# A fused attention, MoE and MLP kernel: the gate factor goes with the scattered rows, and the token order is made once

## The reference

```python
# 1: clustered attention, B=2, H=8, S=768, D=64, 16 clusters
mask = q_assign[:, :, :, None] == k_assign[:, :, None, :]
attn = softmax(where(mask, q @ k.T / sqrt(D), -1e9)); attn_out = attn @ v
x = attn_out.transpose(0, 2, 1, 3).reshape(1536, 512)
# 2: mixture of experts, E=8, F=1024, one expert for a token
logits = x @ w_gate;  e_idx = argmax(logits, axis=1)
gate_w = exp(logits - max)[e_idx] / (sum(exp(logits - max)) + 1e-09)
eom = 1.0 / (1.0 + exp(-(x @ w_output_gate)))
for e in range(E):
    mask = e_idx == e
    h = maximum(x[mask] @ w1[e], 0.0)
    out[mask] = gate_w[mask, None] * eom[mask, e, None] * (h @ w2[e])
# 3: dense MLP, 512 -> 2048 -> 512
h = out @ w_in;  g = h * (1.0 / (1.0 + exp(-1.702 * h)));  result = g @ w_out
```

## Time and profile before

| | |
|---|---|
| median of 3 runs | 777.92 us (777.77 to 779.69) |
| profiled execution, its own time | 778.16 us |
| its span | 776.7 us, 11783 instructions |
| busy: PE, PE weight load | 740.2 us (95%), 629.6 (81%) |
| busy: DVE, ACT, POOL | 420.7 (54%), 375.6 (48%), 177.0 (23%) |
| mean granted clock of TensorE | 0.983 |
| DMA | 61325 packets, 86.28 MB, mean 111 GB/s |

### The profile page before, as it was taken

The page is one execution under the profiler, slowest core; times in us unless marked ns, Lnnn a source line. Parts: engine busy times, 40 slices in busy tenths (PEclk is TensorE's granted clock), DMA queues, the critical chain, the costliest instruction groups (busy, mean ns, idle before and its releaser), DMA issues.

```text
span 776.7 us, 11783 instructions
## 1 busy us (share of the span) xinstructions
PE 740.2 (95%) x4013; PEld 629.6 (81%) x4013; DVE 420.7 (54%) x773; ACT 375.6 (48%) x716; POOL 177.0 (23%) x277
## 2 busy tenths in 40 slices
PE   7899999999999977999999999999999999999994
PEld 5788999988999855778888888788888888888883
DVE  5688798889988854665555555443222212222121
ACT  3687878887788823665566565533011110111010
POOL 5334324334565961101010101100002000010001
PEclk9899999999999997999999999999999999999997
DMA  7875374453748257665546543330001000010001
GB/s 149 208 178 122 79 165 111 106 130 95 184 102 210 86 207 167 253 252 194 187 136 232 208 158 123 122 109 1 0 1 55 0 1 1 0 55 1 0 1 54
DMA packets 61325, 86.28 MB, mean 111 GB/s; under 512 B 32576, under 2 KB 34768, under 8 KB 60752
## 3 DMA queue, kind: packets, MB, share of 16 engines
q1 hardware_dynamic: 54016, 74.80, 34.0%
q0 software_dynamic: 3376, 6.35, 2.3%
q10 hardware_dynamic: 3872, 4.36, 1.8%
HBM read 56.01 MB, written 9.05 MB: 84 GB/s over the span
## 4 chain that ended last, share of the span: by engine, by line
PE 83%; DVE 4%; POOL 3%; issue 2%; ACT 2%; another core or an unknown queue 1%; DMA 1%; ACTq 1%; SPq 0%; DVEq 0%; POOLq 0%
PE ps L1039 17%; PE ps L742 12%; PE ps L821 7%; PE ps L1054 6%; PE ps L1056 6%; PE ps L1055 6%; PE ps L955 4%; PE ps L797 4%; PE ps L793 3%; PE ps L957 3%; PE ps L956 3%; PE ps L968 3%; PE ps L970 3%; PE ps L969 3%; PE ps L808 2%
## 5 line engine op out<-in xcount | busy, mean ns | idle before, releaser
L1314 ACT ACTIVATE g<-ps 128x512 f32<-128x512 f32 x48 | 28.7, 598 | 205.4 <-PE ps L1039 205.4
L1705 DVE CAST gt_h<-g 128x512 fp32r<-128x512 f32 x48 | 20.5, 428 | 179.7 <-ACT g L1314 179.6
L1444 DVE TENSOR_TENSOR pt_l<-ps,pt_h 128x384 fp32r<-128x384 f32 x192 | 98.1, 551 | 31.9 <-ACT pt_h L1147 31.1
L1147 ACT CAST pt_h<-ps 128x384 fp32r<-128x384 f32 x192 | 84.8, 486 | 18.8 <-PE ps L742 18.5
L1400 DVE TENSOR_REDUCE nmax<-ps 128x1 f32<-128x768 f32 x96 | 91.0, 949 | 5.3 <-PE ps L797 5.3
L1123 ACT ACTIVATE probs<-ps,nmax 128x768 f32<-128x768 f32 x96 | 88.4, 920 | 5.6 <-DVE nmax L1400 5.6
L742 PE MATMUL ps<-ident,probs 128*128 128x128 f32 x576 | 84.3, 279 | 3.2 <-ACT probs L1123 1.6
L742 PEld LDWEIGHTS ps<-ident,probs 128*128 128x128 f32 x576 | 66.8, 142 | 12.5 <-DVE pt_l L1444 6.7
L1039 PE MATMUL ps<-x2t_h,wl 128*128 128x512 f32 x192 | 74.9, 390 | 1.5 <-DVE wl L1621 1.5
L1054 PE MATMUL ps<-wh,gt_l 128*128 128x512 f32 x192 | 74.8, 389 | 0.0
L1039 PE MATMUL ps<-x2t_h,wh 128*128 128x512 f32 x192 | 74.7, 389 | 0.0
(11 more groups left out here) (204 smaller groups left out, 1502.4 us busy)
## 6 DMA issues: line engine op xcount, KB each, us to landing
raw<-in_moe_w SPq DMA_DIRECT2D x32, 1024.0 KB, 7.4
ka<-hi_t SPq DMA_DIRECT2D x32, 192.0 KB
raw<-in_moe_w_in SPq DMA_DIRECT2D x4, 1024.0 KB, 5.9
raw<-in_moe_w_out SPq DMA_DIRECT2D x4, 1024.0 KB, 7.2
xg<-xs ACTq DMA_DIRECT2D x15, 256.0 KB, 3.6
qn<-in_q SPq DMA_DIRECT2D x16, 192.0 KB, 3.7
vn<-in_v SPq DMA_DIRECT2D x8, 384.0 KB, 4.2
qa<-hi_t SPq DMA_DIRECT2D x16, 192.0 KB
```

Source lines behind the costliest of these rows:

```text
L1147: nc.scalar.copy(pt_h[g % 2][:, half * GT:(half + 1) * GT, t3 * P:(t3 + 1) * P], ps[:, 4 + half, 0:GQ].rearrange("p (c n) -> p c n", c=GT) ...
L1444: nc.vector.tensor_tensor(pt_l[g % 2][at_p], ps[:, 4 + half, 0:GQ].rearrange("p (c n) -> p c n", c=GT), pt_h[g % 2][at_p].bitcast(F32), AL ...
```

## The change

The gate factor is multiplied into the rows of `xn` before they are scattered to `xs`, and no factor is applied at y. `gate` and `gate_exps` now run once for each of the three stages of tokens, `gain` being one over (1 + exp(-z)) times the sum. The six tiles of batch 0 are scaled by POOL just ahead of each scatter (`rows0_done`), the next three by ACT (`rows1_done`) before `relu(0, 0)`, the last three by DVE (`rows2_done`) before `low(0, 0)`. The scatters of pairs, their zero fill, the loads and copies of them for each tile and `first_info` are gone. The token list is made otherwise: DVE works out each token's dense row (`dense_rows_of_tokens`), and during the MLP, after `gelu_done` 8 (two of which are set at the start), POOL scatters the 12 columns of token numbers, 4 bytes each, to `sorted_token` and loads that once. `place_rows(T)` moves behind the last `add_logits`.

The diff, with declarations of semaphores and tiles and the removed old form of `gate` left out:

```diff
-    row_info = nc.dram_tensor("row_info", (E * REGION + TILE, 2), F32, kind="Internal").ap()
-    sorted_info = nc.dram_tensor("sorted_info", (N + TILE, 2), F32, kind="Internal").ap()
+    sorted_token = nc.dram_tensor("sorted_token", (N, 1), U32, kind="Internal").ap()
...
-            sp.dma_start(row_info.rearrange("(p r) c -> p (r c)", p=P), zeros[:, 0:2 * (E * REGION + TILE) // P]).then_inc(s_fill, 16)
...
+                if t < T:
+                    pool.wait_ge(g_all, 1)
+                    pool.wait_ge(xn_done, PPB * NG)
+                    nc.gpsimd.tensor_scalar(xn[:, t, :], xn[:, t, :], gain[:, t:t + 1], None, ALU.mult).then_inc(rows0_done, 1)
+                    pool.wait_ge(rows0_done, t + 1)
+                elif t < T + GT:
+                    pool.wait_ge(rows1_done, t - T + 1)
+                else:
+                    pool.wait_ge(rows2_done, t - T - GT + 1)
                 nc.gpsimd.indirect_dma_start(xs[:, :], bass.IndirectOffsetOnAxis(pos[:, t:t + 1], 0), xn[:, t, :], None).then_inc(s_disp, 16)
-
-            def place_info(t):
-
-                pool.wait_ge(g_all, t // T + 1)
-                if t == 0:
-                    pool.wait_ge(s_fill, 32)
-                nc.gpsimd.indirect_dma_start(row_info[:, :], bass.IndirectOffsetOnAxis(pos[:, t:t + 1], 0), token_info[:, t, :], None).then_inc(s_info, 16)
...
-            def first_info():
-
-                pool.wait_ge(s_info, 16 * T)
-                nc.gpsimd.dma_start(scale[:, :], row_info[0:TILE, :]).then_inc(sc_in, 16)
-                nc.gpsimd.dma_start(sorted_info[0:TILE, :], row_info[0:TILE, :]).then_inc(s_sorted, 16)
...
-                    if i == PPB + 2 and s in (2, 4, 5, 6, 9, 11):
-                        place_info((2, 4, 5, 6, 9, 11).index(s))
-                    if i == PAIRS - 1 and s == 1:
-                        first_info()
...
-            place_rows(T)
             add_logits(lastg)
-            for t in range(T + 1, NT):
+            for t in range(T, NT):
                 place_rows(t)
-            for t in range(T, NT):
-                place_info(t)
-            pool.wait_ge(s_info, 16 * NT)
-            pool.wait_ge(g_rows, 1)
-            pool.wait_ge(s_sorted, 16)
-            n = pool.value_load(ntiles[0:1, E:E + 1], min_val=E + 1, max_val=MAXT)
-            with pool.Fori(1, n) as p:
-                row = pool.value_load(region_row[0:1, bass.ds(p + 1, 1)], min_val=0, max_val=E * REGION)
-                to = pool.value_load(tile_row[0:1, bass.ds(p + 1, 1)], min_val=0, max_val=N)
-                pool.wait_ge(y_done, p + 1)
-                nc.gpsimd.dma_start(scale[:, :], row_info[bass.ds(row, TILE), :]).then_inc(sc_in, 16)
-                nc.gpsimd.dma_start(sorted_info[bass.ds(to, TILE), :], row_info[bass.ds(row, TILE), :]).then_inc(s_sorted, 16)
-                pool.wait_ge(s_sorted, 16 * p + 16)
-            nc.gpsimd.dma_start(info[:, :, :], sorted_info[0:N, :].rearrange("(n p) c -> p n c", p=P)).then_inc(s_info_in, 16)
-            pool.wait_ge(s_info_in, 16)
-            nc.gpsimd.tensor_copy(row_token[:, :], info[:, :, 0:1].rearrange("p n o -> p (n o)")).then_inc(id_ready, 1)
-            pool.wait_ge(id_ready, 1)
+            pool.wait_ge(g_dense, 1)
+            pool.wait_ge(gelu_done, 8)
+            for t in range(NT):
+                nc.gpsimd.indirect_dma_start(sorted_token[:, :], bass.IndirectOffsetOnAxis(dense_pos[:, t:t + 1], 0), token_id[:, t:t + 1], None).then_inc(s_sorted, 16)
+            pool.wait_ge(s_sorted, 16 * NT)
+            nc.gpsimd.dma_start(row_token[:, :], sorted_token.rearrange("(n p) c -> p (n c)", p=P), allow_slow_non_contiguous=True).then_inc(s_tokens, 16)
+            pool.wait_ge(s_tokens, 16)
...
-            def gate_exps(b):
-
-                act.wait_ge(g_shift, 1 if b == 0 else 3)
-                own = slice(b * T, (b + 1) * T)
-                nc.scalar.activation(zexp[:, own, :], logit[:, own, E:2 * E], ACT.Exp, scale=-1.0).then_inc(g_exp, 1)
+            def gate_exps(st):
+
+                act.wait_ge(g_shift, st + 1)
+                act.wait_ge(g_zsel, st + 1)
+                own = slice(*STAGES[st])
+                nc.scalar.activation(ezs[:, own], esel[:, own], ACT.Exp, scale=-1.0).then_inc(g_exp, 1)
                 nc.scalar.activation(eexp[:, own, :], lsh[:, own, :], ACT.Exp).then_inc(g_exp, 1)
...
+            gate_exps(1)
+            act.wait_ge(g_all, 2)
+            act.wait_ge(xn_done, lastg)
+            for t in range(T, T + GT):
+                nc.scalar.mul(xn[:, t, :], xn[:, t, :], gain[:, t:t + 1]).then_inc(rows1_done, 1)
...
-            def scaled(t):
+            def out_of_expert(t):
                 act.wait_ge(y_ready, t + 1)
-                act.wait_ge(sc_in, 16 * t + 16)
-                nc.scalar.mul(y32[:, :], ps[:, 4, :], scale[:, 1:2]).then_inc(y_done, 1)
-
-            gate_exps(1)
+                nc.scalar.copy(y32[:, :], ps[:, 4, :]).then_inc(y_done, 1)
+
+            gate_exps(2)
...
+            act.wait_ge(s_fill, 16)
...
+                    dve.wait_ge(g_pick, st + 1)
+                    link(nc.vector.tensor_tensor(zexp[:, own, :], logit[:, own, E:2 * E], pick_b[:, own, :], ALU.mult), g_step)
+                    nc.vector.reduce_sum(esel[:, own], zexp[:, own, :], AX.X).then_inc(g_zsel, 1)
...
+            def gate(st):
+
+                own = slice(*STAGES[st])
+                dve.wait_ge(g_exp, 2 * st + 2)
+                link(nc.vector.reduce_sum(esum[:, own], eexp[:, own, :], AX.X), g_step)
+                link(nc.vector.tensor_scalar(esum[:, own], esum[:, own], 1e-9, None, ALU.add), g_step)
+                link(nc.vector.scalar_tensor_tensor(out=esum[:, own], in0=ezs[:, own], scalar=1.0, in1=esum[:, own], op0=ALU.add, op1=ALU.mult), g_step)
+                nc.vector.reciprocal(gain[:, own], esum[:, own]).then_inc(g_all, 1)
+
+            def dense_rows_of_tokens():
+
+                excl = shift[:, 0, :]
+                link(nc.vector.tensor_tensor(shift[:, 1, :], shift[:, 3, :], shift[:, 2, :], ALU.subtract), g_step)
+                link(nc.vector.tensor_tensor(excl, shift[:, 1, :], offset[:, 0, :], ALU.subtract), g_step)
+                nc.vector.tensor_tensor(moved[:, 0:T, :], excl.unsqueeze(1).to_broadcast([P, T, E]), pick_b[:, 0:T, :], ALU.mult)
+                nc.vector.tensor_copy(shift[:, 1, 1:E], shift[:, 0, 1:E])
+                link(nc.vector.tensor_tensor(shift[:, 1, 0:1], shift[:, 0, 0:1], gap[:, 1:2], ALU.subtract), g_step)
+                link(nc.vector.tensor_tensor(moved[:, T:NT, :], shift[:, 1, :].unsqueeze(1).to_broadcast([P, T, E]), pick_b[:, T:NT, :], ALU.mult), g_step)
+                link(nc.vector.reduce_sum(movef[:, :], moved[:, :, :], AX.X), g_step)
+                link(nc.vector.tensor_tensor(movef[:, :], movef[:, :], posf[:, :], ALU.add), g_step)
+                nc.vector.tensor_copy(dense_pos[:, :], movef[:, :]).then_inc(g_dense, 1)
...
+            gate(1)
             choose(2, 0)
             choose(2, 1)
             place(2)
             dve.wait_ge(g_count, 3)
             nc.vector.tensor_copy(filled[:, 1:E], count[:, 2:SEG])
             nc.vector.tensor_tensor(filled[:, 0:1], count[:, 1:2], gap[:, 1:2], ALU.add).then_inc(g_filled, 1)
-            gate(1, 0)
-            gate(1, 1)
+            nc.vector.tensor_copy(shift[:, 2, :], count[:, 1:SEG])
+            link(nc.vector.tensor_tensor_scan(shift[:, 3, :], ones_f[:, 0:E], count[:, 1:SEG], 0.0, ALU.mult, ALU.add), g_step)
+            gate(2)
+            dve.wait_ge(g_all, 3)
+            for t in range(T + GT, NT):
+                nc.vector.tensor_scalar(xn[:, t, :], xn[:, t, :], gain[:, t:t + 1], None, ALU.mult).then_inc(rows2_done, 1)
...
+            dense_rows_of_tokens()
             dense_rows()
```

More of the change, by code:

```diff
@@ L109, in clustered_attention_moe_mlp @@
         least = sb("least", [P, 2, SEG])
-        token_info = sb("token_info", [P, NT, 2])
-        info = sb("info", [P, NT, 2])
+        gain = sb("gain", [P, NT])
+        token_id = sb("token_id", [P, NT], U32)
+        dense_pos = sb("dense_pos", [P, NT], U32)
         row_token = sb("row_token", [P, NT], U32)
@@ L177, in clustered_attention_moe_mlp @@
         esel = at("esel", [P, NT])
+        ezs = at("ezs", [P, NT])
         rank = at("rank", [P, NT, 2, E])
         posf = at("posf", [P, NT])
+        shift = at("shift", [P, 4, E])
+        moved = at("moved", [P, NT, E])
+        movef = at("movef", [P, NT])
         count = at("count", [P, SEG])
@@ L302, in clustered_attention_moe_mlp @@
         xg_in = sem("xg_in")
-        sc_in = sem("sc_in")
+        rows0_done = sem("rows0_done")
+        rows1_done = sem("rows1_done")
+        rows2_done = sem("rows2_done")
+        g_zsel = sem("g_zsel")
+        g_dense = sem("g_dense")
         xt_ready = sem("xt_ready")
@@ L316, in clustered_attention_moe_mlp @@
         x2l_done = sem("x2l_done")
-        id_ready = sem("id_ready")
         h2_ready = sem("h2_ready")
@@ L571, in _ @@
```

(28 more changed lines are left out.)

6 lines of the change are left out of this document (2 added, 4 removed).

## The result

| | before | after |
|---|---|---|
| median in the same job | 778.81 us (4 runs, 777.77 to 779.84) | 767.59 us (4 runs, 767.05 to 768.4) |
| ratio, 95% interval | | 0.9859 [0.9841, 0.9878] |
| span of the profiled execution | 776.7 us | 766.3 us |
| PE busy | 740.2 us (95%) | 737.4 us (96%) |

The kernel is faster by 11.2 us, 1.4%. The forecast was 773.0 with a range of 768.5 to 779.5: the sign was right, the gain was more than twice the 4.9 us foreseen, and the time lies 0.9 us under the range.

The account below looks back on a forecast made before the run. TensorE was taken as the bound, with its waits between the last attention pair and the expert loop to be shortened. Terms -6.2 + 1.0 + 0.3 = -4.9 us gave 773.0 against the median 777.92, range 768.5 to 779.5.

Parts of the forecast that it names:

- POOL's two loads per tile: Loads on POOL for each tile, which the change removes: counted at nothing, hidden behind a tile of 14 us or more.
- part 5: Before tile 1: without six pair scatters, PE's 302.50 becomes 296.3, -6.2 us in all with the earlier parts.
- the clock: TensorE's slow stretch, which covered mostly idle time, will lie more on work: +1.0 us (0 to 1.7).
- part 6: Token order: nine small steps on DVE ahead of low(1, 0), some 2.2 us, mostly covered by idling: +0.3 us.
- hold 2: The 5.59 us wait from 292.80, where PE's signal for the transposes reached ACT late; tied to the pair scatters.
- Rival (a): Before tile 1: PE's late signals come from row scatters and fills, which stay; xg lands as late; 777.8; chance 0.23.
- (b): Before tile 1: both late signals go and xg lands at 294.6, at full clock: another 3 us, 770; chance 0.13.
- Part 1: Last attention pair: dropping first_info's 0.64 + 0.58 us on POOL shrinks PE's 1.29 us stop to 0.1: -1.2 us.
- Parts 2 to 4: From choose to low(0, 0): added steps +0.4, reordered last half batch -0.35, scaling on DVE +0.45 us (to 1.2).
- part 2: In choose on DVE: a multiply and a reduction now stand ahead of xt_l, without cover: +0.4 us.
- Rival (d): Pair 5: POOL's multiplies at 1.35 us each, four ahead of v's halves, give back 5.4 us: 778.4; chance 0.03.
- Rival (c): MLP near 531: small scatters hold TensorE, twelve in a row costing 8.0 us, 781 with the gain kept; chance 0.11.

Follow-up runs that it names:

- the second pair: The kernel before and the kernel after, both unchanged, each profiled a second time: medians 777.21 us and 766.66 us.
- before_again: The kernel before, unchanged, profiled once more: 777.21 us, ratio 0.9996 against the kernel before.
- a_pairs_back: The kernel after, with six scatters of 8 bytes a row put back behind the last row scatter, to an unread tensor: 770.92 us, 0.9943 against before.
- b_pair6_early: The kernel before, with pair 6's six pair scatters at tile slots 1 to 6 instead of 2, 4, 5, 6, 9 and 11: 775.12 us, 0.9987.
- b_fills_later: The kernel before, with the zero fills of regions 1 and 2 issued behind the load of xg for tile 1: 775.8 us, 0.999.
- b_rows_behind: The kernel before, with the first of the last six row scatters behind the last add_logits, not ahead of it: 774.35 us, 0.9975.
- b_first_behind: The kernel before, with first_info's two loads moved from the last attention pair to behind the last row scatter: 772.69 us, 0.9954.
- b_pairs_late: The kernel before, with POOL's last six pair scatters waiting for y_done 2: 781.14 us, 1.0071.
- a_plus32: The kernel after, with 32 small loads of 1 KB more on POOL's queue during the MLP: 769.95 us, 0.9927 against before.
- after_again: The kernel after, unchanged, profiled once more: 766.66 us, 0.9876 against the kernel before.
- a_two_loads: The kernel after, with two small unused loads issued by POOL where first_info stood, in the last attention pair: 768.17 us, 0.9898 against before.
- a_fills_behind: The kernel after, with the zero fills of regions 1 and 2 issued behind the load of xg for tile 1: 767.15 us, 0.9885 against before.

## Why the prediction was wrong, step by step

**What failed: three terms.** First, the sum had no term for the end of the program. "POOL's two loads per tile" stood under nothing, "hidden behind a tile of 14 us or more". Hidden they are, but each of the 32 DMAs that the change takes from POOL comes back in its last drain: -2.6 us. I had read the page up to the plateau of nines, and never the last instruction. With this term the forecast would have been 770.4, still 2.8 us above the measured 767.59.

Second, part 5's two bounds on the load. "Issues at 292 (291 to 294)": it was 290.12. "Between 3.6 us and 7.6, with 4 it is 296": the landing was 2.8. Not all of the 3.3 us between 296.3 and 292.99 belong to this term, for 1.1 of them were there at the mark. The issue gives 0.9: the distance from the last scatter was 2.0 us, my near bound, and I had taken 3. The landing gives 1.2, and it was below my near end, for I took ACT's fifteen loads, which run beside weight loads, as the floor. Between the second profiles the step is 6.8, near my 6.2, but that is luck: it is another start, with the load issued at 292.06 and landed 8.1 later, and no hold.

Third, the clock. I charged +1.0 because the slow stretch would lie on work. In the first pair it did, and cost 2.2 (9.5 at tile 1 became 7.3). In the second pair it was a gain of 1.9: the long stop is what the clock falls in, and a kernel with a shorter stop may not meet it at all. The term's sign was open, and my bounds of 0 to 1.7 shut one side out. Laid beside the second pair, which has no holds, the 6.7 us that my -4.9 lacks of its -11.6 are the clock 2.9, the drain 2.6, tile 1 0.6, part 6 0.3 and 0.3 elsewhere.

**The mechanism.** "If they made hold 2" is refuted as it was put: PE's late signals are absent from before_again, a_pairs_back and the four kernels b_pair6_early, b_fills_later, b_rows_behind and b_first_behind, each with all six pairs in place, and a late signal of 2.3 us is there in the first profile of after, which has none. What makes them isn't settled. What the pairs do is lengthen the load that ends at the same moment, shown in both directions above. My sentence "hold 2 and this load end almost together, so both must move" saved the size by luck: the load alone, without a hold, puts tile 1 at 249.4 from the mark, where with the holds it was 251.1. The nearness in time that I called "no more" than that was indeed no more. Rival (a), the same holds and the same late landing, is refuted, and (b), "both holds go and xg lands at the near bound", 770, was nearest; I gave it 0.13.

**Part 1.** Right in rows: DVE's wait 2.33 to 1.09, the stop gone, tile 0 1.5 us sooner from the mark in b_first_behind. It isn't the only way there: the earlier landing of expert 0's weights does it too.

**Parts 2 to 4.** By the product that waited for `choose(2)` I had 1.15 ahead. Measured from the mark it is 2.1 in the first pair of profiles and 2.0 in the second; the stop for `xt_l` grew by 0.17 us, from 0.19 to 0.36, where part 2 had 0.4. Then `ht_l` comes behind DVE's multiplies (a stop of 0.8) and 1.2 is left in the second pair, where I had 0.7. ACT's multiplies took 0.65 each and delayed nothing; DVE's 0.43 as taken from the cast.

**Part 5, the rest.** The last row scatter's issue ended at 288.16, where I had 289.06; from the mark that is 237.8 against 237.7, so it came when I said. That SP follows it in 1.8 to 2.0 us in all kernels made from after, and in 3.5 to 5.1 in those made from before but one, isn't caused by the pairs (b_pairs_late: 3.5) or the fills. The order with add_logits gives about one of it (b_rows_behind: 2.7); the rest stays open.

**Part 6 and what stood at nothing.** The token order took 1.7 us on DVE and cost nothing; I had +0.3. POOL's multiplies took 1.58 us each, over my far bound of 1.35, 9.5 in all. Rival (d) had the price right and the cover nearly wrong: all seven profiles of kernels made from after have a stop of 0.42 to 0.66 us in pair 5 that none of the seven made from before has, and PE was busy 61.3 to 61.6 of the 62 us of pairs 5 and 6, where before it was 62.00. In the first profile of after it is

```profile
209.85 0.62 PE L782 MATMUL ps<-kb,qb 80*128 80x384 f32 x2 [0.48 <-DMA kb<-onehot_t]
```

It isn't v, as (d) said, but `kb`. The first multiply stands ahead of a split on POOL, and SP's longest wait for that split (`lo_t`) is 10.9 us, where it was 9.4, with the loads of `kb` behind it. That this wait makes the stop is read from the order and not tested. Rival (c) is refuted by the window from 524 to 548: twelve scatters in a row, PE busy throughout.

## What to carry to other kernels

Bytes are a poor price for a DMA: with two to four scatters of 1 KB in front of it a 256 KB load landed 3 to 5.5 us later, and moving two fills of 256 KB from in front of it changed the landing by 0.8 us and by 0.1. A small transfer that nobody waits for can still have a price in whoever's load comes behind it. Count the DMAs that GpSimd issues over the whole program, since the drain at the end charges for each. And profile a kernel twice before an argument is hung on one stop: the two late signals that bounded this profile's stretch were gone in the next execution at the same total time.

## What the runs showed of the hardware

- GpSimd's last drain grows by 80 to 82 ns for each DMA it issued, an indirect scatter or a plain load: 3097 ns with 37, 5706 and 5710 with 69.
- The 256 KB load of `xg` landed in 2.5 to 2.8 us with no scatter of 128 x 8 bytes near it (seven profiles), and in 5.6 to 8.1 with two to four of them ahead of it and the rest of six behind (seven profiles).
- Signals of PE can come late by 2.3 to 5.6 us in one execution and not in the next of the same kernel. In the kernel before, holds of 4.4 and 5.6 us left the span the same within 0.8 us (776.7 and 775.9).
- With stops of like length at the same place the granted clock fell to 0.50 in some executions (a_plus32, 2.78 us, where the transposes took 1.11 us) and stayed at 1.00 in others (after_again, 2.74 us, and a_two_loads, 2.96 us; transposes 0.66 us); it fell after 2.48 us in a_fills_behind and 2.52 in b_pairs_late. In the six kernels that stopped 5.5 to 8.3 us there it fell each time.
